# The exponents of batch 0's next unit on both sides of the state update, normalisation last, and the token matmuls three units behind the attention

## The reference, cut to what matters

```python
m_new = np.maximum(f_gate[:, :, t] + m, i_gate[:, :, t])
f_stab = np.exp(f_gate[:, :, t] + m - m_new)
i_stab = np.exp(i_gate[:, :, t] - m_new)
C = f_stab[..., None, None] * C + i_stab[..., None, None] * np.einsum('bhd,bhe->bhde', vt, kt)
n = f_stab[..., None] * n + i_stab[..., None] * kt
h_tilde = np.einsum('bhde,bhe->bhd', C, qt)
denom = np.maximum(np.abs(np.einsum('bhd,bhd->bh', n, qt)[:, :, None]), 1.0)
y[:, :, t] = sigmoid(o_gate[:, :, t]) * h_tilde / denom
...
h = np.maximum(xt @ w_tok1, 0.0) @ w_tok2      # x is y; xt is x with tokens last
u = x + h.transpose(0, 2, 1)
x = u + np.maximum(u @ w_ch1, 0.0) @ w_ch2
...
out = sigmoid(causal_conv5(x)) * (x @ w_val) @ w_out
```

## Time and profile before

| | us |
|---|---|
| median of 3 runs (lowest, highest) | 289.72 (288.74, 290.57) |
| the profiled execution | 291.4 |
| its span, first to last instruction | 289.3 |
| PE busy | 264.7 (91%) |
| DVE busy | 180.0 (62%) |
| ACT busy | 115.4 (40%) |
| POOL busy | 85.7 (30%) |

### The profile page before, as it was taken

How to read it: one execution, slowest core, us unless ns; L and a number is a source line. 1 busy time by engine, 2 the same in 40 slices (tenths; PEclk the granted TensorE clock), 3 DMA queues, 4 the chain that set the end, 5 groups by cost and what they waited for, 6 DMA issues and landing times.

```text
span 289.3 us, 5204 instructions
## 1 busy us (share of the span) xinstructions
PE 264.7 (91%) x1964; PEld 247.3 (85%) x1964; DVE 180.0 (62%) x401; ACT 115.4 (40%) x212; POOL 85.7 (30%) x102
## 2 busy tenths in 40 slices
PE   0598788999999999999999999999999999999675
PEld 0587677679799999999999997899999999999564
DVE  7988877486878568535866303537653168742991
ACT  2664545488444432443432223322232332232731
POOL 4415578903654553155004000000040000130710
PEclk9999999999999999999999999999999999999988
DMA  7699987664765143220000010000000100000101
GB/s 219 155 274 321 302 265 219 212 198 124 208 189 132 57 142 91 84 68 3 0 0 2 3 66 2 0 0 2 0 2 23 45 1 2 0 2 0 56 13 68
DMA packets 26289, 25.68 MB, mean 89 GB/s; under 512 B 13977, under 2 KB 22009, under 8 KB 26265
## 3 DMA queue, kind: packets, MB, share of 16 engines
q1 hardware_dynamic: 21976, 18.72, 22.2%
q10 hardware_dynamic: 4288, 6.64, 7.1%
HBM read 23.34 MB, written 2.02 MB: 88 GB/s over the span
## 4 chain that ended last, share of the span: by engine, by line
PE 74%; DVE 7%; issue 7%; POOL 5%; ACT 4%; DMA 1%; SPq 0%; ACTq 0%; POOLq 0%; DVEq 0%
PE shared L1172 30%; PE h_ps L1306 22%; PE s_ps L1210 4%; PE hv_ps L1191 2%; PE s_ps L1244 2%; PE hv_ps L1195 2%; DVE gate L1039 2%; PE shared L1271 2%; PE h_ps L1244 2%; POOL qs L597 2%; PE shared L1221 1%; DMA mask_sb<-mask 1%; PE shared L1318 1%; DVE prob L930 1%; PE shared L1256 1%
## 5 line engine op out<-in xcount | busy, mean ns | idle before, releaser
L1104 DVE SCALAR_TENSOR_TENSOR h_lo<-shared,h_hi 128x384 fp32r<-128x384 f32 x48 | 26.5, 557 | 40.2 <-ACT h_hi L824 40.1
L1306 PE MATMUL h_ps<-ch_hi,h_hi 128*128 128x320 f32 x144 | 45.4, 315 | 0.0
L1306 PE MATMUL h_ps<-ch_hi,h_lo 128*128 128x320 f32 x144 | 44.5, 309 | 0.0
L824 ACT ACTIVATE h_hi<-shared 128x384 fp32r<-128x384 f32 x48 | 23.1, 488 | 53.2 <-PE shared L1172 50.1
L1306 PE MATMUL h_ps<-ch_lo,h_hi 128*128 128x320 f32 x144 | 44.3, 308 | 0.0
L1172 PE MATMUL shared<-u_hi,ch_hi 128*128 128x384 f32 x96 | 33.1, 344 | 0.1
L1172 PE MATMUL shared<-u_lo,ch_hi 128*128 128x384 f32 x96 | 32.6, 339 | 0.0
L1172 PE MATMUL shared<-u_hi,ch_lo 128*128 128x384 f32 x96 | 32.5, 339 | 0.0
L1210 PE MATMUL s_ps<-q_in,k_in 128*128 128x128 f32 x192 | 27.1, 300 | 3.9 <-DMA q_in<-qT 3.9
L1210 PEld LDWEIGHTS s_ps<-q_in,k_in 128*128 128x128 f32 x192 | 25.2, 211 | 6.1 <-DMA q_in<-qT 4.5
L1039 DVE SCALAR_TENSOR_TENSOR gate<-x,conv_sb,gate 128x384 f32<-128x384 f32 x44 | 29.0, 668 | 1.0
(11 more groups left out here) (181 smaller groups left out, 550.3 us busy)
## 6 DMA issues: line engine op xcount, KB each, us to landing
G_all<-G_scratch SPq DMA_DIRECT2D x11, 512.0 KB, 5.8
o_sig<-on ACTq DMA_DIRECT2D x2, 960.0 KB, 6.7
k_in<-kT SPq DMA_DIRECT2D x24, 80.0 KB
q_in<-qT SPq DMA_DIRECT2D x24, 80.0 KB
kn_in<-kn SPq DMA_DIRECT2D x12, 160.0 KB, 4.3
v_in<-vn SPq DMA_DIRECT2D x12, 160.0 KB, 4.8
stage<-ch ACTq DMA_DIRECT2D x3, 640.0 KB, 4.3
out<-o_sb SPq DMA_DIRECT2D x12, 160.0 KB, 1.8
```

The lines of the kernel that those rows point to most:

```text
L824: act.activation(h_hi[i % 3][:], ps_of(key)[:, 0:T], ACT.Relu).then_inc(hi_ready, 1)
L1104: took(dve.scalar_tensor_tensor(out=h_lo[i % 3][:], in0=ps_of(key)[:, 0:T], scalar=0.0, in1=h_hi[i % 3][:].bitcast(F32), op0=ALU.max, op1= ...
L1306: last = pe.matmul(h2_ps[t][:, 0:DM], a[:, tile_cols(t)], w[:, f, :], start=(f == 0 and n == 0), stop=(f == FT - 1 and n == 2))
```

## The change

On DVE, in units 1 to 4 of batch 0 (`spread`), the exponents of the next unit no longer stand behind the normalisation. Those of head group 0 come right behind the two products, ahead of the state update, and those of group 1 behind the state update, ahead of the normalisation. On PE, the token matmuls of a unit come one unit earlier, with unit n instead of n+1, and the call behind the last turn is gone. The number of instructions is the same on each engine.

```diff
--- before.py
+++ after.py
@@ -940,6 +940,9 @@
                         dve.wait_ge(exp_ready, w + 1)
                         dve.wait_ge(s_ready, w + 1)
                         dve.tensor_tensor(prob[w % 4][:], s_ps[g][:], prob[w % 4][:], ALU.mult).then_inc(prob_ready, 1)
+                spread = b == 0 and 1 <= n < NC - 1
+                if spread:
+                    exponents(u + 1, (0,))
                 if n < NC - 1:
                     key = ("delta", u)
                     full(dve, key)
@@ -964,6 +967,8 @@
                     else:
                         dve.wait_ge(apart_ready, with_next(u))
                         dve.sem_inc(shared_done[J[key] % 2], 1)
+                if spread:
+                    exponents(u + 1, (1,))
                 if (b, n) in LO_VECTOR_AT:
                     make_lo(dve, *LO_VECTOR_AT[b, n])
                 if n >= 1:
@@ -1005,7 +1010,7 @@
                         took(ins, y_key)
                 if u == 0:
                     columns(1)
-                if n + 1 < NC:
+                if n + 1 < NC and not spread:
                     exponents(u + 1)
 
             def take_h2(q, t):
@@ -1195,9 +1200,9 @@
                             last = pe.matmul(hv_ps[64 * g:64 * g + D1, tile_cols(j)], v_in[v % 3][:, g * HG + j, :],
                                              prob[(2 * v + g) % 4][:, tile_cols(j)], start=(n < 2), stop=True)
                     last.then_inc(hv_ready, 1)
-                if b == 0 and n >= 4:
-
-                    token_hidden(0, n - 4)
+                if b == 0 and n >= 3:
+
+                    token_hidden(0, n - 3)
                 if n < NC:
 
                     pe.wait_ge(q_loaded[k], 32 * (u // 2 + 1))
@@ -1357,7 +1362,6 @@
                     columns(1)
                 else:
                     turn_y(0, n)
-            token_hidden(0, NC - 3)
             for q in range(NQ):
                 if q % 2 == 0:
                     if q > 0:
```

## The result

The changed kernel takes **291.83 us** in the median of 11 runs (290.77 to 294.43), the kernel before 288.92 in 11 (287.68 to 291.33). The ratio is **1.0103, with a 95% interval of 1.0063 to 1.0142**, so the change costs some 3.0 us (1.8 to 4.1). Forecast were 291.6 us and +1.9 us, counted from the median of the three runs known then, 289.72; with eight more runs that median is 288.92.

What follows compares the result with a forecast made beforehand. Landings of v were taken to bound units 1 to 4 of batch 0's attention. A weighing 2.1 us late less 0.2 for token matmuls gave +1.9 us, so a median of 291.6 us from 289.72, range 289.4 to 293.6.

Steps and rivals of the forecast that it cites:

- What bounds the kernel: Attention of batch 0, units 1 to 4: landings of v, one every 6.8 to 7.2 us, set the pace.
- Exponents ahead of the normalisation delay gating and with it the weighing: DVE to POOL, batch 0: weighing of v 2.19, 2.03 and 2.12 us late, not cumulative; taken as 2.1 us slower.
- Token matmuls, a gain of 0.2: PE, end of batch 0's attention: one pair leaves the space before the second transposition; gain 0.1 to 0.4 us, taken 0.2.
- Nothing gives the time back: From 57 us on, each step is released by one that moved with it, so the delay stays.
- The sum of +1.9: Whole kernel: +2.1 for the late weighing, -0.2 for the token matmuls, giving 1.9 us slower.
- the rival without a loss: Weighing in batch 0: earlier G or later v takes up the delay, only the 0.2 gain stays; 289.5 us, chance 0.2.
- The clock rival: PE at 28 to 32 us: thinner work halves TensorE's clock; +3.2 us in all, 292.9 us, chance 0.18.
- main case: Whole kernel: late weighing less the token matmul gain, +1.9 us, median 291.6 us; chance 0.58.
- PE's clock at 1.00 in 28 to 40 us: Sign expected in the profile after: TensorE's granted clock stays full at 28 to 40 us.

Runs made afterwards that it cites:

- e6: Kernel before, with token weights, first two weight pieces and the splitting of these pieces each one unit later; ratio 0.9942 (0.9920 to 0.9963).
- e1: Changed kernel's DVE half only, token matmuls four units behind as in the kernel before; ratio 1.0107 (1.0067 to 1.0148) against the kernel before.
- e3: Changed kernel with batch 0's gating on POOL one unit later, behind qs; ratio 0.9998 (0.9972 to 1.0024) against the kernel before.
- e5: Changed kernel with the normalisation moved back between the two groups of exponents; ratio 1.0064 (1.0032 to 1.0095) against the kernel before.
- e10: Changed kernel again, no edit, for a second trace; its one run took 292.94 us.
- e4: Kernel before again, no edit, for its spread and trace; 12 runs, ratio 0.9985 (0.9959 to 1.0011).
- e9: Kernel before again, no edit, for a further trace; its one run took 288.64 us.
- e11: Changed kernel again, no edit, for a third trace; its one run took 292.26 us.

## Why the prediction was right, and where its size was off

The median, 291.83, lies in the range of 289.4 to 293.6, the change is slower as forecast, and the mechanism is the one that was named. That the forecast 291.6 is so near is partly luck: the forecast of the change was 1.1 us too small, and its base, the median of three runs, 0.8 too high. The forecast also gave 0.73 to a change within 1%; the measured 1.03%, between 0.63 and 1.42, lies on that line and doesn't decide it.

- **What bounds the kernel** (landings of v, then weighing, `kept`, `qs`, output matmuls): right. e6 moved the landings and the time followed, 1.7 us.
- **Exponents ahead of the normalisation delay gating and with it the weighing**: right, by e1 (the whole loss), e3 (none without the order on POOL) and e5 (some with half of the exponents). Forecast lateness of the weighing 2.19, 2.03, 2.12; measured against the same trace 2.05, 1.42, 1.72. DVE ran through what was costed at 4.21 us in 4.12 and 4.13: 23.92 to 28.04, 30.07 to 34.20. The start in unit 1 agrees with the forecast 23.93 by luck, since there it was the product, waiting for slow scores (3.78 us for the 16), and not G, that came last; in e10 G does (a wait of 0.65, start at 24.03). Unit 2 began 0.5 us earlier than in the sum, since G(3) landed at 30.0 and not 30.5; the exponents made in unit 3 then came 0.3 early, at 37.59 and not 37.85.
- **Token matmuls, a gain of 0.2**: right by the traces, 0.18 (13.37 and not 13.55 us from the output matmuls of unit 4 to the mark); not to be seen in the times, 0.9989 (0.9965 to 1.0014). The second transposition did wait for DVE's bank.
- **Nothing gives the time back**: right up to 275 us, 1.53 us there and 1.55 at the mark. Behind that, the first pair lost most of it from sight for another reason (last point).
- **The sum of +1.9**: too small by 1.1, though inside the interval of what was measured. The term that was mis-sized is the delay of the weighing, 2.1. I took it against the landings of one execution, the latest of three: against e4 the weighing of unit 4 is late by 42.88 - 38.75 = 4.1, and against the mean of the three traces of before, 40.04, by 2.8. In the marks, the mean of before is 1.1 us ahead of the trace that I used; the clock puts another 1.0 on the mean of the changed kernel (59.9 and not 58.9). Together with the 1.5 of the first pair these are the 3.6 us between the marks. How the 3.0 us of the runs divide among them is not shown. I named the variation of the landings, but only as a reason for a smaller loss (the rival without a loss, 0.2). It went the other way.
- **The clock rival**: right in place and price (1.3 us on top forecast; 1.6 and 1.1 measured), and wrong in being an alternative with 0.18 and in the sign "PE's clock at 1.00 in 28 to 40 us". It comes on top of the main case, in two of three traces. The clock fell behind a stretch with PE busy 0.83 and 0.89 of 3 us, and stayed with 1.28. One of its grounds was misread: ahead of the slow score matmuls at 18.96 PE had not "hardly worked", it was busy 2.40 of the 3 us from 14 to 17. The clock column reads 1.00 there, though such a matmul took 421 ns and not the 275 of later ones, and in e10, where these scores took 3.39 us, it reads 0.50 from 17 to 20 us. The Trainium skill, "TensorE: Matmul & The Clock Gate", Part 1, has it that the gate keeps a time of its own, so that executions of one kernel differ. They did differ here, but so did their work in the stretch, and no run here tells the two apart.
- **The first pair of profiled executions** hid most of this: 291.4 and 291.97 us. Before had late landings and, from 274.18 on, a last stretch of 11.1 us up to its last matmuls, with the clock at 0.50 on it; that stretch is 9.7 us in the changed kernel and 9.5 to 9.7 in e4, e9, e10 and e11. A fall alone doesn't make it long: in the changed kernel the clock stood at 0.50 from 276 to 279 us, and the stretch was only 0.2 us longer than in e9, where the clock did not fall up to 285. So of the 1.5 us at 275 us only 0.1 was left at the last matmuls.

## What to carry to other kernels

Before you move work ahead of an instruction on an engine with slack, follow who stands behind that instruction on the next engine: here DVE had time to spare, but POOL's gating waited for its last step, and the key of the next unit's chain stood behind the gating. Where a loop is paced by transfers, one trace tells the pace of one execution: take the landings of several before you price a delay against them, since a delay is hidden behind a late landing and laid bare by an early one. And where a wait thins PE's work, look at the granted clock in several traces: here it fell behind that wait in two of three, which added 1.1 and 1.6 us to the delay itself.

## What was not expected of the hardware

- The same program's transfers land at different times in different executions: v(4), sent at 31.1 to 31.4 in all three traces of the kernel before, landed at 38.7, 40.1 and 41.1.
- A fall of TensorE's clock to 1.2 GHz in the middle of a busy kernel, behind a stretch with PE busy 0.83 (e10) or 0.89 (e11) of 3 us. It cost 1.6 and 1.1 us, in which the output matmuls of unit 2 started 0.43 us apart, row by row, and not 0.22.
